# A spectral filter and two feed-forward layers on one core: the first pair's low parts move between two activations, and a copy moves ahead of the high parts

## The chip, the cores and the metric

The kernel runs on one core of one Trainium2 chip. The metric is device microseconds of one execution; the shown time is the median of three runs. Within a core the engines run side by side, each with its own in-order queue of instructions: PE (TensorE, matrix products), DVE (VectorE), ACT (ScalarE), POOL (GpSimd) and SP (SyncE, which here only issues DMAs). They wait for one another on semaphores.

## The reference

```python
def _attn_ref(x, filt_r, filt_i):            # x: 2 x 3008 x 256
    X = np.fft.rfft(x, axis=1)
    Y = X * (filt_r + 1j * filt_i)[None, :, :]
    return np.fft.irfft(Y, n=x.shape[1], axis=1)

def _moe_ref(x, w_in, w_out, alpha):         # 6016 tokens, 256 -> 2048 -> 256
    h = x @ w_in
    g = np.maximum(h, 0.0) + alpha * np.minimum(h, 0.0)
    return g @ w_out

def _moe2_ref(x, w_in, w_out):
    h = np.maximum(x @ w_in, 0.0)
    return h * h @ w_out
```

The spectral filter is followed by the first feed-forward layer, and that by the second. All of it is in fp32.

## The kernel before

The spectral filter of the first batch fills the first 79 us. From then on one long loop runs 2 x 12 x 8 = 192 **slots**. Each layer has 12 groups of 500 or 504 tokens, and a group takes eight slots, one for each pair of 256 hidden features (`FP = 8`). Slot n belongs to group g = n // 8 and has place p = n % 8. The spectral filter of the second batch is woven into the first layer's slots.

Precision comes from splitting: a tensor is written as a high part (fp32r) plus a low part, and a product is the sum of three products of such parts. So an up product is six matmuls for each of two banks (`in_hi` by `w_hi` and `w_lo`, `in_lo` by `w_hi`; lines 890, 891, 895), and the down product, which uses a Strassen-like form with seven products of pieces, is 14 matmuls on the high parts (L916, L918) and seven on the low parts (L928). What one slot does:

- PE: `up(n)` fills the banks `h_ps[0]` and `h_ps[1]`, then `down_high(n-2)` and `down_low(n-2)` (`LAG = 2`) add the pair of two slots ago to the accumulators `m_ps`. `up(n)` may write bank j only when DVE has made product j of slot n-1 (`g_ready`). The low part of a group's first pair is put off: it runs in slot 8g+3, between the two banks of `up` (`late_low`).
- ACT: two activations out of the banks into `g_raw` (L598, Relu), then one copy that makes the high parts `g_hi` of the pair **before** (L507, 1750 or 1764 columns), once POOL has made its last piece.
- DVE: two activation products (L766 in the first layer, L769 in the second), one subtraction for two of the pieces (L773, "differences"), then the low parts `g_lo` of the pair before (L750), once `g_hi` is there.
- POOL: two pieces, T2 (L495) and T4 (L498), both after the differences of the slot.

At the **turn** from group g-1 to g the accumulators of the old group must be emptied before the new group's first pair may write them. `down_low` of the old group's last pair runs in the new group's second slot, 8g+1 (p = 1). In that slot ACT copies the old group's first sum, `m_ps[0]`, into `ct` (L507, `ct<-bank`) after the high parts, and DVE's `combine(g-1)` adds up the rest in four instructions (L735, L739, L742, L744), then makes the low parts of pair 8g. PE's `down_high(8g)`, in the third slot, 8g+2 (p = 2), waits for the sums that it overwrites. There are 23 turns.

Two further things touch DVE near a turn. In slots 51, 59, 67, 75, 83 and 91, which are fourth slots (p = 3) of groups 6 to 11, DVE forms weight sums of the second layer behind the low parts (L675, L678, L680, L682 on `s_raw`). And at p = 5 of the first layer PE has 24 small matmuls of the second transform (`y_group`, L868).

Of the kernel before, what the change touches and what calls it, by code (L numbers as in the profile page):

```python
# [33 lines left out]
FP = FT // 2  # L34
HALF = (252, 250, 250, 252, 250, 250) * BATCH
HMAX = max(HALF)
GMAX = 2 * HMAX
GROUPS = len(HALF)
FIRST = [2 * sum(HALF[:g]) for g in range(GROUPS)]
SLOTS_1 = GROUPS * FP  # L40
LAG = 2
RING = 3
# [9 lines left out]
B12, B11, B22, B21, T1N, T3, T2, T4 = range(8)  # L52
# [99 lines left out]
def spectral_mix_two_ffn(nc, x, filt, w1, w2, alpha, sign, consts, consts_full, const_y, out):  # L152
# [7 lines left out]
    with ctx:  # L160
# [39 lines left out]
        g_raw = sb(g_scope, "g_raw", [P, RING, 8, HMAX])  # L200
# [300 lines left out]
        @block.scalar  # L501
        def _(act):
            for s in (f0.a_out_ready, f0.t_hi_ready, f0.v_ready, f1.a_out_ready, f1.v_ready):
                act.sem_inc(s, PRIME)

            def copy(dst, src):
                return act.activation(dst, src, ACT.Copy)  # L507

            def a_copy(f, u, uses, slot, ps, dma):
                act.wait_ge(f.a_done, done(u))  # L510
                act.wait_ge(f.a_stored[dma], uses * 32 + 32)
                copy(f.a_out[:, slot, :], f.a_ps[ps][0:ROWS, :]).then_inc(f.a_out_ready, 1)

            def t_high(f, n, uses, slot, raw_slot):
                act.wait_ge(f.t_loaded[raw_slot], uses * 16 + 16)
                if n >= f.deep:
                    act.wait_ge(f.spec_done, free(n, f.deep))
                copy(f.t_hi[:, slot, :], f.t_raw[:, raw_slot, :]).then_inc(f.t_hi_ready, 1)

            def filter_copy(n):  # L520
                slot = n % f0.filters
                act.wait_ge(f0.filt_loaded[slot], n // f0.filters * 16 + 16)
                copy(f0.filt[N2:P, slot, :], f0.filt[0:N2, slot, :]).then_inc(f0.filt_ready, 1)

            def swap(n, c):
                act.wait_ge(f1.spec_done, done(n))
                act.wait_ge(f1.im_ready, free(n, 1))
                copy(f1.swapped[c * N2:(c + 1) * N2, :],
                     f1.x_ps[0][(1 - c) * N2:(2 - c) * N2, :]).then_inc(f1.swap_ready, 1)

            def v_copy(f, n, uses, slot, ps):
                act.wait_ge(f.v_done, done(n))
                act.wait_ge(f.v_stored[slot], uses * 16 + 16)
                copy(f.v_out[:, slot, :], f.v_ps[ps][:, :]).then_inc(f.v_ready, 1)

            def w_high(p):
                act.wait_ge(w_sums_ready, p + 1)
                copy(w_hi[:, p, :, :], w_raw[:, p, :, :]).then_inc(w_hi_ready, 1)

            for u in range(A_UNITS):  # L540
                a_copy(f0, u, u // f0.outs, u % f0.outs, u % 2, u % f0.outs // f0.group)

            filter_copy(0)
            for n in range(f0.deep):
                t_high(f0, n, 0, n, n)
            filter_copy(1)
            for n in range(B_UNITS):
                if n + f0.deep < B_UNITS:
                    m = n + f0.deep
                    t_high(f0, m, m // f0.raw, m % f0.deep, m % f0.raw)  # L550
                if n + 2 < B_UNITS:
                    filter_copy(n + 2)
                if n >= 2:
                    v_copy(f0, n - 2, (n - 2) // f0.deep, (n - 2) % f0.deep, n % f0.ring)
            for n in range(B_UNITS - 2, B_UNITS):
                v_copy(f0, n, n // f0.deep, n % f0.deep, n % f0.ring)

            for p in range(EARLY_W):
                w_high(p)
            for s in f0.v_stored:  # L560
                act.wait_ge(s, 16 * (B_UNITS // f0.deep + 1))

            def in_high(g):
                k = g % GROUPS
                for half in range(KD):
                    if g < GROUPS:
                        act.wait_ge(y_done, g * KD + (half + 1))
                        src = y_ps[half][:, 0:2 * HALF[k]]
                    else:
                        act.wait_ge(zin_loaded, k * 32 + 32)  # L570
                        src = zin[:, half, 0:2 * HALF[k]]
                    if g >= 2:
                        act.wait_ge(h_done, (g - 1) * FT)
                    copy(in_hi[:, g % 2, half, 0:2 * HALF[k]], src).then_inc(in_hi_ready, 1)

            in_high(0)
            for n in range(2 * SLOTS_1):
                g, p = divmod(n, FP)
                r, h = n % RING, HALF[g % GROUPS]

                if p == IN_P and g + 1 < 2 * GROUPS:
                    in_high(g + 1)
                if n < SLOTS_1:
                    for u in range(A_UNITS):
                        if A_SLOT[u] + 1 == n:
                            a_copy(f1, u, u // f1.outs, u % f1.outs, u % 2, u % f1.outs)
                    for u in range(B_UNITS):
                        if B_SLOT[u] + 3 == n:
                            v_copy(f1, u, u // f1.deep, u % f1.deep, 0)
                        if B_SLOT[u] + 1 == n:  # L590
                            for c in range(2):
                                swap(u, c)

                for j in range(2):
                    act.wait_ge(h_done, 2 * n + j + 1)
                    if j == 0 and n >= RING:
                        act.wait_ge(down_done, n - RING + 1)
                    act.activation(g_raw[:, r, 2 * j:2 * j + 2, 0:h],  # L598
                                   h_ps[j][:, 0:2 * h].rearrange("p (j d) -> p j d", j=2), ACT.Relu,
                                   scale=-1.0 if n < SLOTS_1 else 1.0).then_inc(relu_ready, 1)  # L600

                if n > 0:
                    q = (n - 1) % RING
                    hq = HALF[(n - 1) // FP % GROUPS]
                    act.wait_ge(t4_ready, n)
                    copy(g_hi[:, q, :, 0:hq], g_raw[:, q, B11:T4 + 1, 0:hq]).then_inc(g_hi_ready, 1)

                if p == LAG - 1 and g > 0:
                    hc = HALF[(g - 1) % GROUPS]
                    act.wait_ge(m_done, 3 * (g - 1) + 1)  # L610
                    if g > 1:
                        act.wait_ge(c_ready, 4 * (g - 1))
                    copy(ct[:, M1, 0:hc], m_ps[0][:, 0:hc]).then_inc(m1_ready, 1)

                if n + EARLY_W < FP:
                    w_high(n + EARLY_W)
                for q in range(FP):
                    if W2_SLOT[q] + 2 == n:
                        act.wait_ge(s_sums_ready, q + 1)
                        if q > 0:  # L620
                            act.wait_ge(s_stored, 32 * q)
                        copy(s_hi[:, :, :], s_raw[:, :, :]).then_inc(s_hi_ready, 1)

            q = (2 * SLOTS_1 - 1) % RING
            act.wait_ge(t4_last, 1)
            copy(g_hi[:, q, :, 0:h], g_raw[:, q, B11:T4 + 1, 0:h]).then_inc(g_hi_ready, 1)
            act.wait_ge(m_done, 3 * (2 * GROUPS - 1) + 1)
            act.wait_ge(c_ready, 4 * (2 * GROUPS - 1))
            copy(ct[:, M1, 0:h], m_ps[0][:, 0:h]).then_inc(m1_ready, 1)

        @block.vector
        def _(dve):
# [122 lines left out]
            for n in range(2 * SLOTS_1):  # L755
# [3 lines left out]
                for j in range(2):  # L759
                    f = 2 * p + j  # L760
                    hidden = h_ps[j][:, 0:2 * h].rearrange("p (j d) -> p j d", j=2)
                    piece = g_raw[:, r, 2 * j:2 * j + 2, 0:h]
                    dve.wait_ge(relu_ready, 2 * n + j + 1)
                    if n < SLOTS_1:

                        dve.scalar_tensor_tensor(out=piece, in0=piece, scalar=rest_sb[:, f:f + 1], in1=hidden,  # L766
                                                 op0=ALU.mult, op1=ALU.add).then_inc(g_ready, 1)
                    else:
                        dve.tensor_tensor(piece, piece, hidden, ALU.mult).then_inc(g_ready, 1)  # L769
                    if j == 0 and p == IN_P and g + 1 < 2 * GROUPS:  # L770
                        in_low(g + 1)
                dve.wait_ge(g_ready, 2 * n + 2)
                dve.tensor_tensor(g_raw[:, r, T1N:T3 + 1, 0:h], g_raw[:, r, B11:B22 + 1, 0:h],  # L773
                                  g_raw[:, r, B12:B12 + 1, 0:h].to_broadcast([P, 2, h]),
# [8 lines left out]

                if p == LAG - 1 and g > 0:
                    combine(g - 1)
                if n > 0:
                    g_low(n - 1)

                if n < SLOTS_1:
# [269 lines left out]
```

## Time and profile before

| | before |
|---|---|
| three runs | 1168.16, 1169.57, 1169.93 us; median 1169.57 |
| the profiled execution | 1168.78 us, its span 1167.0 us |
| mean granted TensorE clock | 0.992 |
| PE busy | 1127.8 us (97%) |
| DVE busy | 977.0 us (84%) |
| ACT busy | 653.5 us (56%) |
| POOL busy | 626.1 us (54%) |

Busy shares are means over the whole program. What a change at one place of a slot is worth is read from the wait that ends last there.

### The profile page before, as it was taken

The numbers are of one execution on the slowest core, as the hardware profiler recorded it, in microseconds if no ns is written. First come the engines' busy times: TensorE is split into PE (matmuls) and PEld (weight loads), VectorE is DVE, ScalarE is ACT, GpSimd is POOL, SyncE is SP. The second block draws the span as 40 slices with busy tenths as digits, with TensorE's granted clock in tenths as the row PEclk, the third lists the DMA queues.
The fourth block names the chain that finished last, engine by engine and source line by source line (L and its number), as shares of the span: only waits on it lengthen the run. The fifth ranks groups of instructions, "written<-read, shape, count | busy, mean of one in ns | idle before, by whom it ended". The sixth has DMA issues, their size and how long they took to land.

```text
span 1167.0 us, 17117 instructions
## 1 busy us (share of the span) xinstructions
PE 1127.8 (97%) x6867; PEld 984.4 (84%) x6867; DVE 977.0 (84%) x1118; ACT 653.5 (56%) x769; POOL 626.1 (54%) x438
## 2 busy tenths in 40 slices
PE   7989999999999999999999999999999999999997
PEld 2556888888889898898898898898889889889886
DVE  0879688897888988888889889888888888888887
ACT  4746556555655555555556555555555555555553
POOL 0606455555566565565565655555546555556553
PEclk9989999999999999999999999999999999999999
DMA  8974353452203312313217801101100110110100
GB/s 247 281 228 117 81 134 87 113 129 73 70 31 115 82 50 82 81 51 81 82 50 238 297 1 36 36 1 36 37 27 10 36 36 1 36 37 1 37 18 18
DMA packets 64304, 93.45 MB, mean 80 GB/s; under 512 B 5344, under 2 KB 50272, under 8 KB 64224
## 3 DMA queue, kind: packets, MB, share of 16 engines
q1 hardware_dynamic: 64224, 92.35, 27.5%
q8 instruction: 54, 0.88, 0.3%
q14 instruction: 26, 0.21, 0.1%
HBM read 55.90 MB, written 36.44 MB: 79 GB/s over the span
## 4 chain that ended last, share of the span: by engine, by line
PE 79%; DVE 10%; ACT 4%; issue 3%; DMA 3%; SPq 0%; POOL 0%; DVEq 0%; ACTq 0%; PEldq 0%; POOLq 0%
PE bank L890 14%; PE bank L895 13%; PE bank L891 13%; PE bank L928 12%; PE bank L918 11%; PE bank L916 11%; DVE g_lo L750 4%; PE bank L868 3%; ACT g_hi L507 2%; DVE ct L735 1%; DVE ct L739 1%; DMA v_rows<-v_out_b 1%; DVE ct L744 1%; PE bank L842 1%; PE bank L836 1%
## 5 line engine op out<-in xcount | busy, mean ns | idle before, releaser
L495 POOL TENSOR_TENSOR g_raw<-g_raw 128x250 f32<-128x250 f32 (+1 forms) x191 | 262.3, 1373 | 454.4 <-DVE g_raw L773 454.4
L598 ACT ACTIVATE g_raw<-bank 128x500 f32<-128x500 f32 (+1 forms) x384 | 226.9, 591 | 402.2 <-PE bank L895 344.0
L750 DVE TENSOR_TENSOR g_lo<-g_raw,g_hi 128x1750 fp32r<-128x1750 f32 (+1 forms) x192 | 419.2, 2184 | 27.0 <-ACT g_hi L507 25.3
L507 ACT ACTIVATE g_hi<-g_raw 128x1750 fp32r<-128x1750 f32 (+1 forms) x192 | 320.3, 1668 | 25.9 <-POOL g_raw L498 22.6
L890 PE MATMUL bank<-in_hi,w_hi 128*128 128x500 f32 (+1 forms) x768 | 309.8, 403 | 17.1 <-DVE g_raw L769 8.6
L918 PE MATMUL bank<-g_hi,w_lo 128*128 128x250 f32 (+1 forms) x1344 | 321.6, 279 | 0.0
L916 PE MATMUL bank<-g_hi,w_hi 128*128 128x250 f32 (+1 forms) x1344 | 321.1, 279 | 0.0
L498 POOL TENSOR_TENSOR g_raw<-g_raw 128x250 f32<-128x250 f32 (+1 forms) x191 | 298.4, 1562 | 15.0
L891 PE MATMUL bank<-in_hi,w_lo 128*128 128x500 f32 (+1 forms) x768 | 298.8, 389 | 0.0
L918 PEld LDWEIGHTS bank<-g_hi,w_lo 128*128 128x128 f32 x1344 | 254.0, 189 | 7.5
L916 PEld LDWEIGHTS bank<-g_hi,w_hi 128*128 128x128 f32 x1344 | 253.8, 189 | 7.4
L895 PE MATMUL bank<-in_lo,w_hi 128*128 128x500 f32 (+1 forms) x768 | 237.2, 390 | 0.0
L928 PE MATMUL bank<-g_lo,w_hi 128*128 128x250 f32 (+1 forms) x1344 | 187.6, 279 | 0.8 <-DVE g_lo L750 0.8
L890 PEld LDWEIGHTS bank<-in_hi,w_hi 128*128 128x128 f32 x768 | 145.0, 189 | 49.8 <-issue 11.2
L766 DVE SCALAR_TENSOR_TENSOR g_raw<-g_raw,rest_sb,bank 128x500 f32<-128x500 f32 (+1 forms) x192 | 137.5, 732 | 52.9 <-ACT g_raw L598 52.5
L928 PEld LDWEIGHTS bank<-g_lo,w_hi 128*128 128x128 f32 x1344 | 172.2, 189 | 2.8 <-DVE g_lo L750 1.0
L895 PEld LDWEIGHTS bank<-in_lo,w_hi 128*128 128x128 f32 x768 | 144.7, 188 | 30.2
L891 PEld LDWEIGHTS bank<-in_hi,w_lo 128*128 128x128 f32 x768 | 144.9, 189 | 25.6 <-issue 4.3
L769 DVE TENSOR_TENSOR g_raw<-g_raw,bank 128x500 f32<-128x500 f32 (+1 forms) x192 | 127.7, 671 | 40.6 <-ACT g_raw L598 40.2
L773 DVE TENSOR_TENSOR g_raw<-g_raw 128x500 f32<-128x500 f32 (+1 forms) x192 | 138.8, 723 | 6.6
L868 PE MATMUL bank<-const_y_sb,vc 96*128 96x94 f32 (+4 forms) x288 | 36.0, 285 | 4.5 <-DMA vc<-v_rows 4.5
L868 PEld LDWEIGHTS bank<-const_y_sb,vc 96*128 96x128 f32 x288 | 35.6, 203 | 4.9 <-issue 4.9
(57 smaller groups left out, 533.8 us busy)
## 6 DMA issues: line engine op xcount, KB each, us to landing
filt_b<-filt SPq DMA_DIRECT2D x36, 256.0 KB, 4.8
vc<-v_rows SPq DMA_DIRECT2D x24, 288.0 KB, 6.2
t_raw_b<-t_rows SPq DMA_DIRECT2D x24, 256.0 KB, 4.5
v_rows<-v_out_b SPq DMA_DIRECT2D x24, 256.0 KB, 3.6
w_rows<-s_hi SPq DMA_DIRECT2D x8, 704.0 KB, 3.1
w_rows<-s_lo SPq DMA_DIRECT2D x8, 704.0 KB, 3.1
w_hi<-w_rows SPq DMA_DIRECT2D x8, 704.0 KB, 5.4
w_lo<-w_rows SPq DMA_DIRECT2D x8, 704.0 KB, 7.1
```

The costliest lines, as they stand in the source:

```text
L495: pool.tensor_tensor(g_raw[:, r, T2, 0:h], g_raw[:, r, B22, 0:h], g_raw[:, r, T1N, 0:h], ALU.add).then_inc(t2_ready, 1)
L498: pool.tensor_tensor(g_raw[:, r, T4, 0:h], g_raw[:, r, B21, 0:h], g_raw[:, r, T2, 0:h], ALU.subtract).then_inc(t4_ready, 1)
L507: return act.activation(dst, src, ACT.Copy)
L598: act.activation(g_raw[:, r, 2 * j:2 * j + 2, 0:h], h_ps[j][:, 0:2 * h].rearrange("p (j d) -> p j d", j=2), ACT.Relu, scale=-1.0 if n < SL ...
L750: dve.tensor_tensor(g_lo[:, q, B11:T4 + 1, 0:h], g_raw[:, q, B11:T4 + 1, 0:h], g_hi[:, q, :, 0:h], ALU.subtract).then_inc(g_lo_ready, 1)
L773: dve.tensor_tensor(g_raw[:, r, T1N:T3 + 1, 0:h], g_raw[:, r, B11:B22 + 1, 0:h], g_raw[:, r, B12:B12 + 1, 0:h].to_broadcast([P, 2, h]), AL ...
L890: pe.matmul(o, w_hi[:, p, 2 * j + k, :], in_hi[:, g % 2, k, cols], start=(k == 0), stop=False)
L891: pe.matmul(o, w_lo[:, p, 2 * j + k, :], in_hi[:, g % 2, k, cols], start=False, stop=False)
L895: mm = pe.matmul(o, w_hi[:, p, 2 * j + k, :], in_lo[:, g % 2, k, cols], start=False, stop=(k == KD - 1))
L916: pe.matmul(o, w_hi[:, p, tile, :], g_hi[:, q, piece - B11, 0:h], start=(first and side == 0), stop=False, skip_group_check=True)
L918: pe.matmul(o, w_lo[:, p, tile, :], g_hi[:, q, piece - B11, 0:h], start=False, stop=False, skip_group_check=True)
L928: mm = pe.matmul(o, w_hi[:, p, tile, :], g_lo[:, q, piece, 0:h], start=False, stop=last, skip_group_check=True)
```

## The change

Two moves, with no instruction added or taken away. On ACT the copy of the old group's first sum goes from behind the high parts to ahead of them, in every second slot of a group. On DVE the low parts of a group's first pair, which stood behind `combine` in the second slot, go into the third slot, between its two activation products.

```diff
@@ scalar engine, in slot n
-                if n > 0:
-                    q = (n - 1) % RING
-                    hq = HALF[(n - 1) // FP % GROUPS]
-                    act.wait_ge(t4_ready, n)
-                    copy(g_hi[:, q, :, 0:hq], g_raw[:, q, B11:T4 + 1, 0:hq]).then_inc(g_hi_ready, 1)
-
                 if p == LAG - 1 and g > 0:
                     hc = HALF[(g - 1) % GROUPS]
                     act.wait_ge(m_done, 3 * (g - 1) + 1)
                     if g > 1:
                         act.wait_ge(c_ready, 4 * (g - 1))
                     copy(ct[:, M1, 0:hc], m_ps[0][:, 0:hc]).then_inc(m1_ready, 1)
+
+                if n > 0:
+                    q = (n - 1) % RING
+                    hq = HALF[(n - 1) // FP % GROUPS]
+                    act.wait_ge(t4_ready, n)
+                    copy(g_hi[:, q, :, 0:hq], g_raw[:, q, B11:T4 + 1, 0:hq]).then_inc(g_hi_ready, 1)
@@ vector engine, in slot n
                     if j == 0 and p == IN_P and g + 1 < 2 * GROUPS:
                         in_low(g + 1)
+                    if j == 0 and p == LAG and g > 0:
+
+                        g_low(n - LAG)
@@
                 if p == LAG - 1 and g > 0:
                     combine(g - 1)
-                if n > 0:
+                elif n > 0:
                     g_low(n - 1)
```

DVE at the turn to group 8, from the second slot's activation products to the fourth slot's weight sums. Before:

```order
L766 SCALAR_TENSOR_TENSOR g_raw<-g_raw,rest_sb,bank 128x2x250 x2
L773 TENSOR_TENSOR g_raw<-g_raw 128x2x250
L735 TENSOR_TENSOR ct<-bank,ct 128x2x250
L739 TENSOR_TENSOR ct<-bank,ct 128x2x250
L742 TENSOR_TENSOR ct<-bank,ct 128x250
L744 TENSOR_TENSOR ct<-bank,ct 128x2x250
L750 TENSOR_TENSOR g_lo<-g_raw,g_hi 128x7x250
L766 SCALAR_TENSOR_TENSOR g_raw<-g_raw,rest_sb,bank 128x2x250 x2
L773 TENSOR_TENSOR g_raw<-g_raw 128x2x250
L750 TENSOR_TENSOR g_lo<-g_raw,g_hi 128x7x250
```

The same place in the changed kernel, from `combine`'s first instruction on:

```order
L735 TENSOR_TENSOR ct<-bank,ct 128x2x250
L739 TENSOR_TENSOR ct<-bank,ct 128x2x250
L742 TENSOR_TENSOR ct<-bank,ct 128x250
L744 TENSOR_TENSOR ct<-bank,ct 128x2x250
L766 SCALAR_TENSOR_TENSOR g_raw<-g_raw,rest_sb,bank 128x2x250
L750 TENSOR_TENSOR g_lo<-g_raw,g_hi 128x7x250
L766 SCALAR_TENSOR_TENSOR g_raw<-g_raw,rest_sb,bank 128x2x250
L776 TENSOR_TENSOR g_raw<-g_raw 128x2x250
L750 TENSOR_TENSOR g_lo<-g_raw,g_hi 128x7x250
```

The first `g_lo` (of the group's first pair) now stands behind the third slot's first product; everything behind the second product is as it was.

ACT at the same turn, from the second slot's activations on. Before:

```order
L598 ACTIVATE g_raw<-bank 128x2x250 x2
L507 ACTIVATE g_hi<-g_raw 128x7x250
L507 ACTIVATE ct<-bank 128x250
L598 ACTIVATE g_raw<-bank 128x2x250 x2
L507 ACTIVATE g_hi<-g_raw 128x7x250
```

And in the changed kernel:

```order
L598 ACTIVATE g_raw<-bank 128x2x250 x2
L507 ACTIVATE ct<-bank 128x250
L507 ACTIVATE g_hi<-g_raw 128x7x250
L598 ACTIVATE g_raw<-bank 128x2x250 x2
L507 ACTIVATE g_hi<-g_raw 128x7x250
```

The copy of the old group's first sum and the high parts of the new group's first pair have changed places. The instructions and their order on PE, POOL and SP are the same.

## Rows read from the trace of the kernel before

**Rows 1.** The profile's page, chain that ended last: shares of the span by engine

```profile
PE 79%; DVE 10%; ACT 4%; issue 3%; DMA 3%; SPq 0%; POOL 0%; DVEq 0%; ACTq 0%; PEldq 0%; POOLq 0%
```

**Rows 2.** The waits of PE: who waited for whom, total us, times, longest

```profile
PE bank L890 <- DVE g_raw L769: 8.6, 12, 1.2
PE bank L890 <- DVE g_raw L766: 8.5, 10, 1.7
```

**Rows 3.** Timeline of PE: start, us, engine, line; in brackets the idle time before

```profile
350.33 0.49 PE L890 MATMUL bank<-in_hi,w_hi 128*128 128x500 f32 x1 [1.53 <-DVE g_raw L766]
...
662.94 0.46 PE L890 MATMUL bank<-in_hi,w_hi 128*128 128x504 f32 x1 [1.17 <-DVE g_raw L769]
705.29 0.49 PE L890 MATMUL bank<-in_hi,w_hi 128*128 128x500 f32 x1 [0.70 <-DVE g_raw L769]
...
795.82 0.39 PE L890 MATMUL bank<-in_hi,w_hi 128*128 128x504 f32 x1
...
801.02 0.39 PE L890 MATMUL bank<-in_hi,w_hi 128*128 128x504 f32 x1
...
826.79 0.39 PE L890 MATMUL bank<-in_hi,w_hi 128*128 128x500 f32 x1
...
1127.57 0.50 PE L890 MATMUL bank<-in_hi,w_hi 128*128 128x500 f32 x1 [0.67 <-DVE g_raw L769]
```

**Rows 4.** Timeline of DVE at the turn to group 8

```profile
479.20 0.68 DVE L773 TENSOR_TENSOR g_raw<-g_raw 128x500 f32<-128x500 f32 x1
480.25 0.68 DVE L735 TENSOR_TENSOR ct<-bank,ct 128x500 f32<-128x500 f32 x1 [0.37 <-ACT ct L507]
...
482.60 1.97 DVE L750 TENSOR_TENSOR g_lo<-g_raw,g_hi 128x1750 fp32r<-128x1750 f32 x1
484.49 1.37 DVE L766 SCALAR_TENSOR_TENSOR g_raw<-g_raw,rest_sb,bank 128x500 f32<-128x500 f32 x2
485.89 0.68 DVE L773 TENSOR_TENSOR g_raw<-g_raw 128x500 f32<-128x500 f32 x1
...
491.60 2.23 DVE L750 TENSOR_TENSOR g_lo<-g_raw,g_hi 128x1750 fp32r<-128x1750 f32 x1 [0.41 <-ACT g_hi L507]
493.76 0.82 DVE L675 SCALAR_TENSOR_TENSOR s_raw<-s_raw 128x128 f32<-128x128 f32 x1
...
495.35 1.38 DVE L766 SCALAR_TENSOR_TENSOR g_raw<-g_raw,rest_sb,bank 128x500 f32<-128x500 f32 x2
```

**Rows 5.** Timeline of ACT at the turn to group 8

```profile
478.30 1.66 ACT L507 ACTIVATE g_hi<-g_raw 128x1750 fp32r<-128x1750 f32 x1
479.85 0.37 ACT L507 ACTIVATE ct<-bank 128x250 f32<-128x250 f32 x1
481.61 0.59 ACT L598 ACTIVATE g_raw<-bank 128x500 f32<-128x500 f32 x1 [1.39 <-PE bank L895]
...
489.90 1.67 ACT L507 ACTIVATE g_hi<-g_raw 128x1750 fp32r<-128x1750 f32 x1 [0.19 <-POOL g_raw L498]
```

**Rows 6.** Timeline of POOL at the turn to group 8, fourth slot

```profile
491.27 0.73 POOL L495 TENSOR_TENSOR g_raw<-g_raw 128x250 f32<-128x250 f32 x1 [1.40 <-DVE g_raw L773]
492.08 2.35 POOL L498 TENSOR_TENSOR g_raw<-g_raw 128x250 f32<-128x250 f32 x1
```

**Rows 7.** Timeline of PE at the turn to group 8

```profile
479.24 0.97 PE L928 MATMUL bank<-g_lo,w_hi 128*128 128x250 f32 x7
...
482.77 0.27 PE L916 MATMUL bank<-g_hi,w_hi 128*128 128x250 f32 x1
...
484.27 0.28 PE L918 MATMUL bank<-g_hi,w_lo 128*128 128x250 f32 x1
485.27 0.49 PE L890 MATMUL bank<-in_hi,w_hi 128*128 128x500 f32 x1 [0.72 <-DVE g_raw L766]
...
496.51 0.39 PE L890 MATMUL bank<-in_hi,w_hi 128*128 128x500 f32 x1
```

**Rows 8.** Timeline of DVE at the turn to group 15, fifth slot

```profile
798.21 0.67 DVE L769 TENSOR_TENSOR g_raw<-g_raw,bank 128x504 f32<-128x504 f32 x1
```

## The prediction

> **What bounds the kernel now.** I read the chain that ended last first: PE holds 79% of it [rows 1], so only time in which PE waits is worth anything. The waits of PE come next. In the long loop two kinds matter, both in front of the first `up` matmul of a slot (L890) and both for DVE's activation product of the slot before: 8.6 us in 12 waits in the second layer and 8.5 us in 10 in the first [rows 2]. The timeline says where they stand. The twelve of the second layer are its twelve turns: the first took 1.17 us, the other eleven about 0.68 each [rows 3]. Of the ten in the first layer one, at the turn to group 5, took 1.53 us [rows 3]; six, at the turns to groups 6 to 11, took 0.70 to 0.76 like the 0.72 of group 8 [rows 7]; the other three, 2.6 us together, lie in the first group, which the change doesn't touch. At the turns to groups 1 to 4 PE has more of the spectral filter's matmuls and doesn't wait.
>
> The turn to group 8 shows why. PE's last high matmul of the third slot starts at 484.27, so the next `up` would be due one pitch of 0.12 later, at 484.39. It starts at 485.27 [rows 7]. It waits for the third slot's first product, which DVE starts at 484.49, because the low parts of the group's first pair stand ahead of it from 482.60 on [rows 4]. Its input was there long before: the activation started at 481.61 and took 0.59 [rows 5]. PE needs those low parts only in the fourth slot. So DVE's order is what PE waits for, not DVE's amount of work.
>
> **What a turn costs.** More than the idle time in the bracket, since the pipeline starts anew and the bracket counts from a modelled end. From the turn to group 13 to that of group 23 the starts go from 705.29 to 1127.57: ten groups of 42.23 us. Six slots without a turn go from 795.82 to 826.79, 5.16 each, and eight of them are 41.29 [rows 3]. A turn thus costs 0.94 us for an idle of about 0.68, which is idle plus 0.26. In the second layer that is 8.6 + 12 x 0.26 = 11.7 us. In the first it is 1.53 + 0.26 = 1.8 for group 5 and 6 x (0.72 + 0.26) = 5.9 for the six others. Together 19.4 us: the most that this change can give by these waits.
>
> **The change, part by part, at the turn to group 8.**
>
> The copy on ACT. It waits for the first of the seven low matmuls of the old group. That one starts at 479.24 [rows 7] and a matmul of this size takes 0.28, so with a handover of 0.03 the copy can start at 479.55, 0.30 before its present 479.85 [rows 5]. DVE, which now sits idle for 0.37 before L735, and whose differences end at 479.88, starts `combine` at 479.95 and not 480.25 [rows 4]. Nothing is paid for that on ACT: the high parts, now from 478.30, go to 479.82 and end 1.66 later, at 481.48 [rows 5]. Queued behind them are the third slot's activations, and the first of these starts at 481.61 anyhow. The reader of the high parts on PE comes at 482.77 [rows 7], so 1.29 us are left of their cover. If that cover were gone, each further microsecond would cost PE one.
>
> The low parts on DVE. `combine` takes 2.35 us (480.25 to 482.60 [rows 4]) and now ends at 482.30. The first product follows at once, its input having been ready since 482.20, and is done by 483.0. PE wants it at 484.39: 1.4 us to spare, and the stall is gone. Then come the low parts, 482.95 to 484.92. PE wants them after its first bank of `up` of the fourth slot, whose six matmuls are about 1.36 us, so at 485.75: 0.8 to spare. The second product follows at 484.85, done at 485.5, and PE wants it after the seven low matmuls, at 486.57: 1.1 to spare. The differences start 0.29 earlier than their 485.89. POOL and SP keep their order, and no DMA is issued elsewhere.
>
> What is late next. PE is now 0.98 us ahead of the old time, and DVE only 0.3. In the second layer this is covered: the fifth slot's first product starts at 798.21 and takes 0.67 [rows 8], and PE wants it at 801.02 [rows 3], 2.1 us later; less 0.94 leaves 1.2. In groups 6 to 11 of the first layer it isn't. There the weight sums stand ahead of the fifth slot's first product: the sums start at 493.76, the product at 495.35 [rows 4], and PE takes it at 496.51 [rows 7]. With its length of about 0.66 and a handover of 0.06 the spare is only 0.43.
>
> How much earlier is that product? The low parts ahead of it wait for high parts, those for POOL, and POOL for the third slot's differences. So they could start 0.30 earlier, at 491.30 instead of 491.60. But POOL's two pieces of the fourth slot, now at 491.27 and 492.08 [rows 6], follow PE and come 0.95 earlier: the second runs from 491.13 to 491.86. The rows show what such a meeting costs. The low parts that meet nothing took 1.97 us; those that started at 491.60, while POOL's piece ran until 492.00, took 2.23, and ended 1.83 after it [rows 4, 6]. So the new ones end at 491.86 + 1.83 = 493.69, only 0.14 earlier than now. The sums and the product follow: product done and handed over at 495.93, wanted at 496.51 - 0.98 = 495.53. PE waits 0.40 and starts anew for 0.1: 0.5 us at each of six turns, 3.0 us. The bounds of this term are 0 (if POOL's piece isn't met) and 0.98 a turn (if DVE gains nothing and more is given back); 0.5 is nearest to the row of the meeting.
>
> The Trainium skill, page "SBUF — State Buffer", section "SBUF: two separate sides", says that DVE with two SBUF inputs and GpSimd share a port pair under an exclusive lock that is held for the whole instruction. By that rule the low parts would run their full 1.97 after 491.86 and gain nothing; the term would be 3.8 us and not 3.0. The rows show 1.83 after the lock's end, so they agree within 0.14 us.
>
> At the turn to group 5 DVE comes late by itself. The low parts of its first pair move back by one product, 0.65 us, and may now be late for PE; no row shows their spare at the new time. The bounds are 0 and 0.65, and I take 0.3.
>
> The sum: 19.4 - 3.0 - 0.3 = **16.1 us**. The profiled execution, 1168.78 us, would become 1152.7. It lies 0.8 under the median of the runs, so the median of 1169.57 becomes **1153.4**.
>
> **The rivals.**
>
> The port isn't met. DVE's low parts of groups 6 to 11 win the race, which I reckon at only 0.17 us (491.30 against 491.13), or the spare is larger than I think. Then they take 1.97 us and end at 493.3, PE doesn't wait in the fifth slot, and the gain is 19.1 us: 1150.5. For it: the narrow margin. Against it: the whole of POOL's chain follows PE, and PE's 0.98 is sure if the stall goes.
>
> The stall only moves. DVE proves full through the whole turn, the time saved in the third slot is asked back in the fourth or fifth in both layers, and only the copy's 0.30 is left: 19 x 0.30 = 5.7 us, 1163.9. For it: no work is taken off DVE. Against it: the 1.2 us of spare in the second layer.
>
> Nothing changes. The waits are put down to the product by the profile, and another release behind it comes at the same time: 1169.6. Against it: in rows 7 and 4 the start of PE follows the end of the first product by hundredths.
>
> Slower. On ACT the high parts of the new group's first pair, and behind them the two activations of the third slot, now stand behind a wait for PE's low matmul. The mechanism decides at 1.29 us: if the copy starts later than 480.84, `down_high` of the third slot waits for the high parts, at every one of the 23 turns. If it waited for the last of the seven matmuls, 0.7 us later, there would still be no loss. At 2.2 us late PE would lose 0.9 a turn, 21 us against a gain of up to 19, with the third slot's products late as well: about 1173. For it: the wait is new in front of that work. Against it: activations follow their matmul closely everywhere.
>
> **How the numbers follow.** The forecast has 0.60, the port not met 0.19, the moved stall 0.09, no change 0.05, slower 0.07. A measurement of this kernel can tell about 0.2%, 2.3 us, from no change; so faster has 0.88, same 0.05 and slower 0.07. The range takes in the bounds of the first layer's term (13.2 to 19.1 us of gain, 1150.5 to 1156.4) with a microsecond below, and reaches up to 1160, where half of a moved stall would lie. It leaves out about 0.16.
>
> **What the profile of the changed kernel would show.** The waits of PE for L766 and L769 fall from 17.1 us to about 5: the three of the first group, 2.6, and six of 0.2 to 0.5 in front of the sixth slot's `up` of groups 6 to 11. No wait is left in front of the fourth slot's `up`. The groups of the second layer come every 41.3 us. The copy on ACT shows a wait for PE (L928) that it didn't have, and ends 0.3 earlier against PE. The low parts in the fourth slot of groups 6 to 11 take near 2.4 us with POOL's second piece just ahead. I would be wrong if PE waited for g_hi in the third slot (the copy too late), for g_lo or the second product in the fourth, or if waits for the first product stayed in the second layer.

## The result and the profile after

The changed kernel takes 1151.49 us (median of six runs, 1149.56 to 1153.12) against 1169.89 (six runs, 1168.16 to 1171.66). The ratio is 0.9843, 95% interval 0.983 to 0.9856, so 16.8 to 19.9 us are gained, 18.4 by the medians. Forecast were 1153.4 us, 16.1 us less than before.

| | before | after |
|---|---|---|
| median | 1169.89 us | 1151.49 us |
| profiled execution, span | 1168.78, 1167.0 us | 1153.12, 1151.3 us |
| PE busy | 1127.8 us (97%) | 1124.8 us (98%) |
| DVE busy | 977.0 us (84%) | 963.9 us (84%) |
| POOL busy | 626.1 us (54%) | 597.3 us (52%) |

The profiled execution of after is the slowest of its six runs. Its part ahead of group 1, which the change doesn't touch, took 136.6 us and that of before 133.7. The comparison is therefore made from group 1's first slot on. Busy time by windows of before and of after: length, then busy us of PE, PEld, DVE, ACT, POOL, then PE's granted clock:

```profile
133.73:1167.00 1033.27, 1011.42 (x6412) 908.03 (x6410) 890.35 (x972) 577.40 (x671) 578.94 (x403) 1.00 0.22 65
```
```profile
136.62:1151.30 1014.68, 1007.13 (x6412) 906.90 (x6410) 877.30 (x972) 580.05 (x671) 550.23 (x403) 1.00 0.23 66
```

The same instructions take 18.6 us less, with a granted clock of 1.00, the full level, in both. DVE and POOL are also busy for less, 13 and 29 us, though nothing was taken from them. That hint comes back below.

The chain that ended last and the waits of PE, after (the lines of `up` are now L893, L894, L898, those of the high and low down matmuls L919, L921 and L931):

```profile
PE 90%; issue 3%; DVE 3%; DMA 2%; POOL 1%; ACT 1%; DVEq 0%; SPq 0%; PEldq 0%; POOLq 0%; ACTq 0%
```
```profile
PE bank L893 <- DVE g_raw L766: 2.3, 2, 1.7
```

PE's share of the chain went from 79% [rows 1] to 90%. The 22 waits of [rows 2] have become two: one of 1.69 us in the first group, and one of 0.63 that is new. The first group, which the change doesn't touch, had three such waits before; this execution shows one of them, and the profile of a second measurement of the same kernel ("after, again" below) shows all three, 2.6 us. So the two that are missing here are no gain of the change. At the turns to groups 5 to 23 none is left.

The turn to group 8 on DVE, after (start, us, engine, line), which answers to [rows 4]:

```profile
478.52 0.68 DVE L776 TENSOR_TENSOR g_raw<-g_raw 128x500 f32<-128x500 f32 x1
479.29 0.68 DVE L735 TENSOR_TENSOR ct<-bank,ct 128x500 f32<-128x500 f32 x1
...
481.63 0.73 DVE L766 SCALAR_TENSOR_TENSOR g_raw<-g_raw,rest_sb,bank 128x500 f32<-128x500 f32 x1
482.28 1.98 DVE L750 TENSOR_TENSOR g_lo<-g_raw,g_hi 128x1750 fp32r<-128x1750 f32 x1
484.17 0.73 DVE L766 SCALAR_TENSOR_TENSOR g_raw<-g_raw,rest_sb,bank 128x500 f32<-128x500 f32 x1
484.93 0.68 DVE L776 TENSOR_TENSOR g_raw<-g_raw 128x500 f32<-128x500 f32 x1
...
490.64 2.34 DVE L750 TENSOR_TENSOR g_lo<-g_raw,g_hi 128x1750 fp32r<-128x1750 f32 x1 [1.12 <-ACT g_hi L507]
492.90 0.28 DVE L675 SCALAR_TENSOR_TENSOR s_raw<-s_raw 128x128 f32<-128x128 f32 x1
...
493.95 1.37 DVE L766 SCALAR_TENSOR_TENSOR g_raw<-g_raw,rest_sb,bank 128x500 f32<-128x500 f32 x2
```

On ACT and on PE, after, which answer to [rows 5] and [rows 7]:

```profile
478.87 0.38 ACT L507 ACTIVATE ct<-bank 128x250 f32<-128x250 f32 x1 [1.16 <-PE bank L931]
479.15 1.67 ACT L507 ACTIVATE g_hi<-g_raw 128x1750 fp32r<-128x1750 f32 x1
480.93 0.59 ACT L598 ACTIVATE g_raw<-bank 128x500 f32<-128x500 f32 x1
```
```profile
478.56 0.97 PE L931 MATMUL bank<-g_lo,w_hi 128*128 128x250 f32 x7
...
482.08 0.27 PE L919 MATMUL bank<-g_hi,w_hi 128*128 128x250 f32 x1
...
483.59 0.28 PE L921 MATMUL bank<-g_hi,w_lo 128*128 128x250 f32 x1
483.71 0.39 PE L893 MATMUL bank<-in_hi,w_hi 128*128 128x500 f32 x1
...
494.85 0.39 PE L893 MATMUL bank<-in_hi,w_hi 128*128 128x500 f32 x1
```

The low parts (482.28) stand between the two products (481.63, 484.17). The first product is done at 482.36, and PE takes it at 483.71, one pitch after its last high matmul at 483.59, with no bracket. The copy starts 0.31 us after the first low matmul's start (478.56, 478.87), DVE starts `combine` without a wait, and the high parts end at 480.82, 1.26 us before their reader at 482.08.

### The profile page after: what moved, and what is told of

It reads as the page before. It is cut to its first block, busy times and chain, and to the rows that moved or that the text cites. A ratio compares the mean times of both kernels' runs of the same rounds, so it can differ in the third digit from the quotient of the medians.

```text
span 1151.3 us, 17117 instructions
## 1 busy us (share of the span) xinstructions
PE 1124.8 (98%) x6867; PEld 983.8 (85%) x6867; DVE 963.9 (84%) x1118; ACT 656.6 (57%) x769; POOL 597.3 (52%) x438
## 4 chain that ended last, share of the span: by engine, by line
PE 90%; issue 3%; DVE 3%; DMA 2%; POOL 1%; ACT 1%; DVEq 0%; SPq 0%; PEldq 0%; POOLq 0%; ACTq 0%
PE bank L893 15%; PE bank L898 15%; PE bank L894 15%; PE bank L921 13%; PE bank L919 13%; PE bank L931 13%; PE bank L871 3%; DMA v_rows<-v_out_b 1%; PE bank L820 1%; PE bank L845 1%; PE bank L839 1%; DVE g_lo L750 1%; DMA t_raw_b<-t_rows 1%; DVE g_raw L766 0%; DMA vc<-v_rows 0%
## 5 line engine op out<-in xcount | busy, mean ns | idle before, releaser
L495 POOL TENSOR_TENSOR g_raw<-g_raw 128x250 f32<-128x250 f32 (+1 forms) x191 | 278.4, 1457 | 467.3 <-DVE g_raw L776 467.3
L921 PE MATMUL bank<-g_hi,w_lo 128*128 128x250 f32 (+1 forms) x1344 | 321.8, 279 | 0.0
L919 PE MATMUL bank<-g_hi,w_hi 128*128 128x250 f32 (+1 forms) x1344 | 321.2, 279 | 0.0
L893 PE MATMUL bank<-in_hi,w_hi 128*128 128x500 f32 (+1 forms) x768 | 309.5, 403 | 2.4 <-DVE g_raw L766 2.3
L894 PE MATMUL bank<-in_hi,w_lo 128*128 128x500 f32 (+1 forms) x768 | 299.8, 390 | 0.0
L921 PEld LDWEIGHTS bank<-g_hi,w_lo 128*128 128x128 f32 x1344 | 254.1, 189 | 7.5
L919 PEld LDWEIGHTS bank<-g_hi,w_hi 128*128 128x128 f32 x1344 | 253.8, 189 | 7.4
L498 POOL TENSOR_TENSOR g_raw<-g_raw 128x250 f32<-128x250 f32 (+1 forms) x191 | 251.4, 1316 | 15.0
L898 PE MATMUL bank<-in_lo,w_hi 128*128 128x500 f32 (+1 forms) x768 | 237.8, 391 | 0.0
L931 PE MATMUL bank<-g_lo,w_hi 128*128 128x250 f32 (+1 forms) x1344 | 187.8, 279 | 0.8 <-DVE g_lo L750 0.8
L931 PEld LDWEIGHTS bank<-g_lo,w_hi 128*128 128x128 f32 x1344 | 172.2, 189 | 3.0 <-DVE g_lo L750 1.3
L893 PEld LDWEIGHTS bank<-in_hi,w_hi 128*128 128x128 f32 x768 | 145.7, 190 | 30.7 <-issue 7.2
L898 PEld LDWEIGHTS bank<-in_lo,w_hi 128*128 128x128 f32 x768 | 145.2, 189 | 30.4
L894 PEld LDWEIGHTS bank<-in_hi,w_lo 128*128 128x128 f32 x768 | 145.5, 189 | 26.2 <-issue 4.5
L776 DVE TENSOR_TENSOR g_raw<-g_raw 128x500 f32<-128x500 f32 (+1 forms) x192 | 132.2, 689 | 6.6
```

Source lines behind the costliest of these rows:

```text
L495: pool.tensor_tensor(g_raw[:, r, T2, 0:h], g_raw[:, r, B22, 0:h], g_raw[:, r, T1N, 0:h], ALU.add).then_inc(t2_ready, 1)
L498: pool.tensor_tensor(g_raw[:, r, T4, 0:h], g_raw[:, r, B21, 0:h], g_raw[:, r, T2, 0:h], ALU.subtract).then_inc(t4_ready, 1)
L893: pe.matmul(o, w_hi[:, p, 2 * j + k, :], in_hi[:, g % 2, k, cols], start=(k == 0), stop=False)
L894: pe.matmul(o, w_lo[:, p, 2 * j + k, :], in_hi[:, g % 2, k, cols], start=False, stop=False)
L898: mm = pe.matmul(o, w_hi[:, p, 2 * j + k, :], in_lo[:, g % 2, k, cols], start=False, stop=(k == KD - 1))
L919: pe.matmul(o, w_hi[:, p, tile, :], g_hi[:, q, piece - B11, 0:h], start=(first and side == 0), stop=False, skip_group_check=True)
```

## The experiments

All but "copy alone" are built on the changed kernel. Each ratio is to runs of the kernel before that were taken beside the experiment (medians of 1169.73 to 1170.28 us), so it can differ a little from the quotient of the medians shown. The last two columns are read from the starts of the slots in each one's profiled execution: from slot 8 to slot 96 (the first layer behind its first group), and from slot 96 to slot 191 (the second layer).

| kernel | median, us | ratio to before, interval | slots 8 to 96 | slots 96 to 191 |
|---|---|---|---|---|
| before | 1169.89 | | 513.1 | 502.2 |
| after | 1151.49 | 0.9843, 0.983 to 0.9856 | 506.7 | 490.6 |
| after, again | 1152.14 | 0.9844, 0.9825 to 0.9863 | 506.6 | 490.6 |
| low parts alone | 1155.57 | 0.9865, 0.9845 to 0.9885 | 508.7 | 490.7 |
| copy alone | 1163.74 | 0.9937, 0.9922 to 0.9952 | 511.4 | 498.3 |
| POOL later | 1155.05 | 0.9871, 0.9854 to 0.9888 | 509.8 | 490.5 |
| ACT late by 0.8 | 1154.87 | 0.9868, 0.9848 to 0.9887 | 510.0 | 490.6 |
| ACT late by 1.7 | 1171.10 | 1.0002, 0.9989 to 1.0014 | 517.2 | 498.7 |
| low parts behind the second product | 1162.95 | 0.9935, 0.9919 to 0.9951 | 511.4 | 497.2 |
| low parts behind the differences | 1177.75 | 1.0062, 1.0044 to 1.008 | 516.2 | 505.9 |
| input low parts behind slot 94 | 1152.98 | 0.984, 0.9819 to 0.986 | 506.4 | 490.7 |
| input low parts in slot 95 | 1150.55 | 0.9832, 0.9812 to 0.9852 | 505.6 | 490.5 |

### Each of the two moves alone

The low parts alone: the copy goes back behind the high parts.

```diff
-                if p == LAG - 1 and g > 0:
-                    ...
-                    copy(ct[:, M1, 0:hc], m_ps[0][:, 0:hc]).then_inc(m1_ready, 1)
-
                 if n > 0:
                     ...
                     copy(g_hi[:, q, :, 0:hq], g_raw[:, q, B11:T4 + 1, 0:hq]).then_inc(g_hi_ready, 1)
+
+                if p == LAG - 1 and g > 0:
+                    ...
+                    copy(ct[:, M1, 0:hc], m_ps[0][:, 0:hc]).then_inc(m1_ready, 1)
```

> The changed kernel with the copy on ACT back behind the high parts; only the move of the low parts is left. Theory (DVE's order is what PE waited for): combine starts 0.3 us later, the third slot's first product still comes 1.0 us before PE wants it, the second product 0.7 us before. No wait in front of the fourth slot's up. In groups 6 to 11 the fifth slot's first product has 0.11 us to spare in the changed kernel, so there PE may wait some 0.2 us at six turns: 1151.5 to 1154 us, at least 15 of the 18 us kept. Rival (the copy's 0.3 us is a good part of the gain, by each turn): 1157 us or more, with waits for L766 and L769 back in front of the fourth slot.

The second layer keeps all of its gain (490.7 us against 490.6). The first loses 2.0 us. Its slots 52, 60 and so on take about 0.2 us more than the ordinary slot (5.32 against 5.15 at group 8), and the turn to group 5 0.3 more. The time of 1155.6 is above the 1151.5 to 1154 of the theory, while the starts of the slots lie inside it.

The copy alone, on the kernel before: the diff of ACT's part and nothing else.

> The kernel before with only the copy on ACT moved ahead of the high parts. Theory: combine starts 0.3 us earlier at the turns of groups 6 to 11 and 13 to 23, 0.7 at group 12, and nothing at group 5, where DVE is late by itself. PE's wait at a turn falls from about 0.7 to about 0.4 us: 17 x 0.3 + 0.7 = 5.8 us gained, 1164 us. DVE's wait for the copy (9.7 us in all before L735) is nearly gone. Rival (the copy made the gain and the low parts' place is immaterial): 1152 us. Rival (the copy's wait holds up ACT): 1170 us or more.

DVE at the turn to group 8, and the waits of PE:

```profile
480.18 0.68 DVE L735 TENSOR_TENSOR ct<-bank,ct 128x500 f32<-128x500 f32 x1
...
482.52 1.97 DVE L750 TENSOR_TENSOR g_lo<-g_raw,g_hi 128x1750 fp32r<-128x1750 f32 x1
484.41 1.37 DVE L766 SCALAR_TENSOR_TENSOR g_raw<-g_raw,rest_sb,bank 128x500 f32<-128x500 f32 x2
```
```profile
PE bank L890 <- DVE g_raw L766: 6.8, 11, 1.6
PE bank L890 <- DVE g_raw L769: 4.6, 12, 0.4
```

L735 starts with no wait for the copy, and the twelve waits of the second layer shrink from 8.6 us in all [rows 2] to 4.6: 0.3 a turn, with 0.7 at group 12. The time is 1163.7 us, where 1164 was expected. So the copy alone gives about 6 us. Under the other move it is worth only the 2.0 us in the first layer, since elsewhere PE had that much to spare already. The two gains don't add.

### What became of the loss expected in the first layer

The forecast took 0.5 us a turn off at groups 6 to 11. After has no wait there. The rows show why: the low parts of the fourth slot end at 492.98, as early as reckoned (493.69 on the clock of before, which reads 0.68 more at this turn: 484.39 there is 483.71 here), but the weight sums behind them take 1.05 us (492.90 to 493.95) and not 1.59 (493.76 to 495.35 [rows 4]). All of the difference is in the first, L675: 0.28 us now, 0.82 before [rows 4]. POOL at that place, after, to be held against [rows 6]:

```profile
489.60 0.73 POOL L495 TENSOR_TENSOR g_raw<-g_raw 128x250 f32<-128x250 f32 x1 [0.70 <-DVE g_raw L776]
490.41 0.73 POOL L498 TENSOR_TENSOR g_raw<-g_raw 128x250 f32<-128x250 f32 x1
```

Before, POOL's second piece was asked for at 492.08 while the low parts ran, took 2.35 us and ended at 494.43; L675 was asked for at 493.76 and ended at 494.58. After, the piece is done at 491.14, ahead of it all. The test puts the meeting back and changes nothing else: POOL makes its first piece twice in those six slots.

```diff
                 pool.wait_ge(t13_ready, n + 1)
+                if n in (51, 59, 67, 75, 83, 91):
+                    pool.tensor_tensor(g_raw[:, r, T2, 0:h], g_raw[:, r, B22, 0:h], g_raw[:, r, T1N, 0:h],
+                                       ALU.add).then_inc(again, 1)
+                    pool.wait_ge(again, n // FP - 5)
                 pool.tensor_tensor(g_raw[:, r, T2, 0:h], g_raw[:, r, B22, 0:h], g_raw[:, r, T1N, 0:h],
                                    ALU.add).then_inc(t2_ready, 1)
```

> The changed kernel in which POOL makes its first piece twice in slots 51, 59, 67, 75, 83 and 91 (fourth slots of groups 6 to 11), so that its second piece comes 0.8 us later and asks after DVE's low parts have started, as in the kernel before. Theory (the first weight sum L675 is blocked by POOL's second piece, which itself was blocked by the low parts): that piece takes 2.3 us and not 0.73, L675 takes 0.82 us and not 0.28, and PE, which has 0.11 us to spare there, waits 0.4 in front of the sixth slot's up and loses 0.5 at each of six turns: 3 us, 1154.5 us. Rival (L675 is short for another reason, such as the time of its load): L675 stays at 0.28 us and the time at 1151.5.

POOL, DVE and PE of this kernel at the turn to group 8 (its lines are shifted: L503 is POOL's second piece, L755 the low parts, L680 the first weight sum, L898 `up`):

```profile
489.34 0.73 POOL L500 TENSOR_TENSOR g_raw<-g_raw 128x250 f32<-128x250 f32 x1
490.15 2.35 POOL L503 TENSOR_TENSOR g_raw<-g_raw 128x250 f32<-128x250 f32 x1
```
```profile
489.57 2.34 DVE L755 TENSOR_TENSOR g_lo<-g_raw,g_hi 128x1750 fp32r<-128x1750 f32 x1 [1.12 <-ACT g_hi L512]
491.83 0.82 DVE L680 SCALAR_TENSOR_TENSOR s_raw<-s_raw 128x128 f32<-128x128 f32 x1
...
493.42 1.38 DVE L771 SCALAR_TENSOR_TENSOR g_raw<-g_raw,rest_sb,bank 128x500 f32<-128x500 f32 x2
```
```profile
494.20 0.49 PE L898 MATMUL bank<-in_hi,w_hi 128*128 128x500 f32 x1 [0.28 <-DVE g_raw L771]
```

The piece takes 2.35 us again, the first sum 0.82, and PE waits. Slots 8 to 96 take 3.2 us more than after, about 0.5 at each of six turns, and the second layer is unchanged. The expected 3 us and 0.82 were met. The chain is shown: POOL's piece behind the low parts, the sum behind POOL's piece, PE behind the sum.

### Where the low parts may stand

One step later: behind the second product. Two steps later: behind the differences as well.

```diff
-                    if j == 0 and p == LAG and g > 0:
+                    if j == 1 and p == LAG and g > 0:
 
                         g_low(n - LAG)
```
```diff
-                    if j == 0 and p == LAG and g > 0:
-
-                        g_low(n - LAG)
...
+                if p == LAG and g > 0:
+                    g_low(n - LAG)
                 if p == LAG - 1 and g > 0:
                     combine(g - 1)
```

Two steps later was run first.

> The changed kernel with the first pair's low parts one step later still, behind the third slot's second product and differences. PE wants them 0.82 us after their end in the changed kernel; here they come 0.7 + 0.6 = 1.3 us later, behind a product and the differences. Theory: PE waits 0.5 us for g_lo in front of L931 in the fourth slot, 0.6 with the new start, at 19 or more turns, less what the earlier differences give back: 1160 to 1164 us. Rival (anywhere behind the first product is as good): 1151.5.

DVE and PE of this kernel at the turn to group 8 (L930 is the low down matmul):

```profile
484.34 0.72 DVE L766 SCALAR_TENSOR_TENSOR g_raw<-g_raw,rest_sb,bank 128x500 f32<-128x500 f32 x1
485.62 0.73 DVE L766 SCALAR_TENSOR_TENSOR g_raw<-g_raw,rest_sb,bank 128x500 f32<-128x500 f32 x1 [0.55 <-ACT g_raw L598]
486.39 0.68 DVE L773 TENSOR_TENSOR g_raw<-g_raw 128x500 f32<-128x500 f32 x1
486.98 4.39 DVE L750 TENSOR_TENSOR g_lo<-g_raw,g_hi 128x1750 fp32r<-128x1750 f32 x2
```
```profile
489.01 1.08 PE L930 MATMUL bank<-g_lo,w_hi 128*128 128x250 f32 x7 [1.07 <-DVE g_lo L750]
```

The wait is the one expected, for `g_lo`, but of 1.07 us and not 0.5, and the kernel is slower than before: 1177.8 us, not 1160 to 1164. The expectation missed a term. With the low parts out of the way the second product isn't ready: it waits 0.55 us for its activation. Low parts start 2.6 us after the first product (484.34, 486.98) and in the changed kernel 0.65 (481.63, 482.28), so they are 2.0 us later and not 1.3. The next run tells this apart from a meeting with POOL. (The 4.39 us are two low parts; the first took 1.97, so it was late and not long.)

> The changed kernel with the first pair's low parts one step later, behind the third slot's second product and ahead of the differences. In the run with them behind the differences they started 2.0 us later than in the changed kernel, 0.55 of it idle, since the second product had to wait for its activation, and PE waited 1.07 us. Theory (that idle time is what the place between the two products fills): the low parts start 0.72 us earlier than in that run, still 1.3 later than in the changed kernel, PE waits about 0.35 us and loses 0.6 at each of 22 turns: 13 us, 1165 us. Rival (it was the meeting with POOL's first piece behind the differences that made them late, not the idle time): no wait, 1152 us.

```profile
486.00 1.07 PE L931 MATMUL bank<-g_lo,w_hi 128*128 128x250 f32 x7 [0.35 <-DVE g_lo L750]
```

PE waits 0.35 us, as worked out (0.30 at the turns of the second layer), and the kernel takes 1163.0 us, 2 less than expected. So the place between the two products is good for two reasons: the first product gets out, and the low parts fill a gap of half a microsecond in which DVE would sit idle for the second activation.

### The cover on ACT

The rival on the slower side was that the high parts behind the copy's wait come too late. Their cover was reckoned at 1.29 us and read at 1.26. Two kernels copy three, then all seven pieces of the high parts twice in the second slots, which puts the high parts off.

```diff
                     act.wait_ge(t4_ready, n)
+                    if p == LAG - 1 and g > 0:
+                        copy(g_hi[:, q, 0:3, 0:hq], g_raw[:, q, B11:B11 + 3, 0:hq]).then_inc(again, 1)
+                        act.wait_ge(again, g)
                     copy(g_hi[:, q, :, 0:hq], g_raw[:, q, B11:T4 + 1, 0:hq]).then_inc(g_hi_ready, 1)
```

> The changed kernel in which ACT, at every turn, copies three of the seven pieces of the high parts once more between the copy of the first sum and the high parts: about 0.8 us more. In the changed kernel the high parts of a group's first pair end 1.27 us before PE wants them, and the third slot's first product 1.34 before. Theory (a threshold near 1.27): high parts end 0.5 us before PE wants them, the first product has 0.7 to spare, and the second layer loses nothing. In groups 6 to 11 of the first layer the fifth slot has only 0.11 to spare and loses up to 0.7 a turn: 1152 to 1156 us. Rival (every microsecond in front of the high parts costs PE one): 22 x 0.8 = 18 us, 1169.

> As the run with 0.8 us, but all seven pieces are copied once more, 1.67 us. Theory (a threshold near 1.27): PE waits for the high parts 0.4 us in front of L919 in the third slot, and then for the third slot's products, in all 0.5 to 0.9 us at each of 22 turns: 1163 to 1171 us. Rival (ACT has more cover than the 1.27 us): within 2 us of the run with 0.8.

With 0.8 us the second layer takes 490.6 us as after; only the first loses, 3.3 us, at the fifth slots. With 1.67 us both lose. ACT and PE of the latter at the turn to group 8 (L923 is the high down matmul), and the sum of such waits:

```profile
481.52 3.37 ACT L508 ACTIVATE g_hi<-g_raw 128x1750 fp32r<-128x1750 f32 x2
484.79 1.05 ACT L599 ACTIVATE g_raw<-bank 128x500 f32<-128x500 f32 x2
```
```profile
484.94 0.38 PE L923 MATMUL bank<-g_hi,w_hi 128*128 128x250 f32 x1 [0.33 <-ACT g_hi L508]
PE bank L923 <- ACT g_hi L508: 7.1, 22, 0.3
```

PE waits 0.33 us at 22 turns, and the second layer loses 8.1 us, 0.68 a turn. The whole gain of the change is gone (ratio 1.0002). Below the cover ACT's time was free in the second layer, above it each turn pays, and it pays more than the excess: 1.67 us are 0.41 beyond the 1.26.

### The one new wait

After has one wait for DVE that before hadn't, in slot 95, the last of the first layer. PE, DVE and POOL there:

```profile
639.33 0.49 PE L893 MATMUL bank<-in_hi,w_hi 128*128 128x500 f32 x1 [0.63 <-DVE g_raw L766]
```
```profile
633.10 2.56 DVE L750 TENSOR_TENSOR g_lo<-g_raw,g_hi 128x1750 fp32r<-128x1750 f32 x1 [1.14 <-ACT g_hi L507]
...
636.22 2.40 DVE L718 TENSOR_TENSOR in_lo<-zin,in_hi 128x504 fp32r<-128x504 f32 x2
```
```profile
636.21 1.28 POOL L454 TENSOR_TENSOR s_lo<-s_raw,s_hi 128x512 fp32r<-128x512 f32 x1
```

Slot 94's second product stands behind the input low parts of the second layer (L718), whose two instructions take 2.40 us beside POOL's low parts of the weights. At the other groups the two take 1.3, and at this place before they took 1.80. DVE there, before:

```profile
637.36 1.98 DVE L750 TENSOR_TENSOR g_lo<-g_raw,g_hi 128x1750 fp32r<-128x1750 f32 x1
...
639.90 1.80 DVE L718 TENSOR_TENSOR in_lo<-zin,in_hi 128x504 fp32r<-128x504 f32 x2
```

Slot 95 starts on PE at 641.71 before and at 637.17 after. Against that start, L718 comes 0.86 us later after (0.95 ahead of it, and 1.81 before), because the low parts in front of it start 0.28 later and take 2.56 us and not 1.98; and L718 itself takes 0.60 longer. So the second product (638.55 after, 641.63 before) is 1.46 us later, of which L718's own length is the smaller part. Slot 95 takes 6.09 us and took 5.14 before: it costs 0.95 us. Two kernels move L718: behind slot 94's own low parts, then between the products of slot 95. The diff is that of the second.

```diff
-                    if j == 0 and p == IN_P and g + 1 < 2 * GROUPS:
+                    if j == 0 and p == (IN_P + 1 if g + 1 == GROUPS else IN_P) and g + 1 < 2 * GROUPS:
                         in_low(g + 1)
```

> The changed kernel in which DVE makes the second layer's first input low parts (L718, from zin) behind the low parts of slot 94 and not between its two activation products. Theory: the one wait for DVE that the changed kernel has behind the first group, 0.63 us in front of the second bank of slot 95, goes, with 0.9 us of PE's time: 1150.6 us. Rival: the wait turns into one for the input low parts in slot 96 or for the low parts of slot 93, and the time stays at 1151.5.

> The changed kernel in which the second layer's first input low parts (L718 from zin) stand between the two activation products of slot 95 instead of slot 94, where POOL isn't at work. Theory: L718 takes 1.3 us for two and not 2.4, PE waits neither in slot 95 nor in front of slot 96, and 0.9 us are won against the changed kernel: 1151 us, to be seen in the starts of the slots rather than in the time. Rival: the wait moves once more.

Behind slot 94's low parts, L718 still meets POOL (2.35 us), the products of slot 95 come late, and slot 95 takes 5.81 us, with 0.50 of idle in front of slot 96: the rival was right, the wait had moved. In slot 95:

```profile
636.34 1.81 DVE L718 TENSOR_TENSOR in_lo<-zin,in_hi 128x504 fp32r<-128x504 f32 x2
```

It meets POOL here too, for 0.5 us, so the 1.3 wasn't reached, but PE no longer waits: slot 95 takes 5.14 us, and slots 8 to 96 take 505.6 us, 1.0 less than after. The ratio of 0.9832 is the lowest measured. Its interval overlaps that of the changed kernel, so only the starts of the slots show the gain.

## Why the prediction was right, and where it wasn't

- **What bounds.** Right: PE waited for the first product because of DVE's order. With the low parts moved alone, not one of the waits for a first product in front of the fourth slot's `up` is left in groups 5 to 23. The groups of the second layer come every 41.30 us after, 42.23 before, as forecast.
- **The cost of a turn, idle plus 0.26.** Right. Slots 66 and 67 took 11.31 us before and 10.32 after (479.37 to 489.69), 0.99 less. The second layer was to gain 11.7 us and gained 11.6.
- **The copy's 0.30.** Right: L735 starts 0.77 us after the differences (478.52, 479.29) with no wait in between, and the copy alone gave 5.7 us by the starts of the slots and 6 by the medians, where its own expectation had 5.8.
- **The spare of the moved low parts and products.** Reckoned 1.4, 0.8 and 1.1 us for the first product, the low parts and the second product; read 1.34, 0.82 and 1.00.
- **The low parts that meet POOL.** Right: reckoned to end 1.83 us after POOL's piece, at about 2.4 us of length; read 2.34, and an end of 492.98, 1.84 after 491.14. The narrow race of 0.17 us was won by POOL as reckoned.
- **The fifth slot of groups 6 to 11, 3.0 us.** Wrong, and this is the term that failed. The step was "the sums and the product follow": the sums were carried over with their old 1.59 us. But L675's 0.82 was itself a meeting with POOL's second piece, which the change moves away. The rows were there: 0.82 us for L675 [rows 4], and a piece of 2.35 us that starts at 492.08 [rows 6] and so ends at 494.43, behind the 493.76 at which the sum starts. The sums lost 0.54 us, which left PE 0.11 to spare. With the meeting restored the term is 3.2 us, close to the 3.0; as the kernel stands it is 0. The rival that PE wouldn't wait there (19.1 us less, 1150.5) had the size of this term right, though not by its mechanism: the meeting that it left out did take place.
- **Group 5, 0.3 us off.** Slots 42 and 43 took 12.08 us before and 10.44 after: 1.64 gained, 1.5 forecast. The low parts were just late, as supposed: slot 43 took 0.1 us more than its like.
- **Slot 95.** Not foreseen: 0.95 us lost.
- **The price beyond ACT's cover.** Put too low, though no term of the sum hung on it: a microsecond of PE for each microsecond beyond the 1.29. With 0.41 beyond the measured 1.26, a turn of the second layer lost 0.68.

The first layer's sum thus becomes 7.7 - 0.2 - 0.95 = 6.6 us against 6.5 read, and not 4.4. With the 11.6 of the second layer and 0.4 at the end, that is 18.5, against the 18.6 of the windows. The 0.4 is no effect of the change: the second profile of the changed kernel ends 17.9 us after the start of slot 191, as before, and from slot 8 on it is 18.1 us shorter. That the total came out only 2.3 us from the forecast is in part luck, since the loss in slot 95 hid a third of the 3.0 us that didn't come.

The rule of the Trainium skill that was weighed (page "SBUF — State Buffer", section "SBUF: two separate sides": one exclusive lock for DVE with two SBUF inputs and a GpSimd instruction that reads SBUF, held for the whole instruction) also covers what was missed. By it L675, with both inputs in SBUF, must wait for POOL's piece to end, and the trace agrees within 0.13 us: L675 ended at 494.58, 0.15 us after the piece, and takes 0.28 us when nothing is in its way. I applied the rule to the instruction that moved and not to its neighbour.

## What to carry to other kernels

Where the bounding engine waits for a short result behind a long one on the same queue, and needs the long one later, change their order; the slack of each is read from the starts of its reader, and a gap in which the engine waits for its next input is the best place for the long one. Before old durations are carried into a new order, look at each for an instruction that takes longer than its like: it may be in a meeting that the change undoes or makes. And the gains of two moves that shorten the same wait don't add; reckon the second with the first in place.

## What the runs showed of the hardware

- A wait of POOL's can be handed on to DVE's next instruction: low parts 2.34 us (1.98 alone), POOL's piece 2.35 (0.73 alone), a small sum 0.82 (0.28 alone). The changed kernel's 18.6 us on PE go along with 29 us less of POOL's and 13 less of DVE's busy time, for the same instructions. Of POOL's pieces (L495, L498), 171 took over 1.5 us before and 151 after, and 20 times the 1.6 us between the two lengths is about the 29. So part of the busy time was blocked time, not work.
- A wait of PE costs more than the bracket says. Over the turns of the second layer, 0.32 us of idle before a high matmul went with 0.68 lost, 0.30 before a low one with 0.55, and 0.68 before an `up` with 0.94. Part of it is the bracket itself, which counts from the end of a record of 0.28 us where the next matmul would start 0.12 after the last (484.27 to 485.27 in [rows 7] is 0.88 more than that pitch, for a bracket of 0.72); 0.1 more is the first matmul behind the wait, 0.49 us and not 0.39.
